# A planned order in which GpSimd waits for VectorE at their shared SBUF port

## The chip, the cores and the metric

The kernel runs on one core of a Trainium2 chip. The metric is device time of one execution in microseconds (us), the median of several runs; lower is better. The engines are called TensorE (PE, its weight loads PEld), VectorE (DVE), ScalarE (ACT), GpSimd (POOL) and SyncE (SP), as in the profile.

## The reference, cut to what matters

Linear attention with a decaying state (batch 4, 8 heads, 768 steps, head size 48), then a Fourier mix of its output and a two-layer network with weights 384 x 1536 and 1536 x 384:

```python
for t in range(S):
    cur = einsum('bhd,bhe->bhde', u * k[t], v[t])
    y[t] = einsum('bhd,bhde->bhe', r[t], state + cur)
    state = w[t] * state + einsum('bhd,bhe->bhde', k[t], v[t])
...
u = x + real(fft(fft(x, axis=1), axis=2))     # x: y with the heads side by side
un = (u - mean(u)) / sqrt(var(u) + 1e-06)
out = u + relu(un @ w_ch1) @ w_ch2
```

## The kernel before

**The work.** Each of the 4 batches is cut into 6 chunks of 128 steps. A chunk of attention loads `in_w`, `in_k`, `in_r` and `in_v`, takes the logarithm of w (`lb`, ScalarE), sums it up with TensorE, takes exponentials (`e`), scales r and k with them (`rkh`), transposes these (`rkt`), multiplies them into a masked matrix (`ah`), and adds the state's part; `rk` = r\*k\*u, its row sums `dc` and `vtd` = v\*`dc` carry the current step; `x` is the sum (L1060). `vb` is v in bf16 (L969). Then a batch is folded (`sd`, `xf`), mixed by TensorE (`hcs`, `hcr`, `uf`), normalised (`bst`, `agg`, `un`), and passed through the network in two halves: W1 gives `ht` (L1188, evicted by L1193 or L1195), W2 gives `osb` (L1206, L1210), which is stored. The first three pairs of chunks of batch 0 use `attention2`, the other chunks `attention`. The attention of one batch runs beside the network of the one before it.

**The order.** Every operation is made once by `g.op(...)` and has a number, in the order of the calls. Many operations can run on two or three engines (`alts`). `ORDER` gives each engine the list of numbers that it executes, in that order; an operation that is in GpSimd's list runs on GpSimd. Five operations of the list that are spoken of below: 555 is `vb` of chunk 3 of batch 1 (L969), 536 and 537 are two `sd` of batch 1, 538 is an `xf` that reads both, 780 and 781 are `rk` of chunk 5 of batch 1; 252 and 253 are the two requests for W1 and W2.

**The planner.** `schedule` walks the five lists with fixed durations (`alts`), and gives each operation a planned start and end, and each TensorE tile its PSUM bank. It never makes the order. Operations with `o.port` (all on GpSimd but DMA requests, and those of VectorE that are marked `port=("dve",)`: tensor-tensor operations, casts and the like from SBUF to SBUF) are taken as users of one shared port: in the plan, none starts before the last one of the other engine has ended. `emit` then writes the instructions: an instruction waits on semaphores for the operations in its `deps`, which are true data dependences and reuse of buffers and banks. The port has no part in `deps`, so nothing in the program holds two users of the port apart.

Most SBUF tensor-tensor operations come out of the helper `tt` and have its line, L527; `ts` is L531 and L532, `act` L541, `evict` L550 (ScalarE) and L551 (VectorE).

Of the kernel before, what the change touches and what calls it, by code (L numbers as in the profile page):

```python
# [58 lines left out]
    "act": (  # L59
# [12 lines left out]
    "dve": (  # L72
# [15 lines left out]
    "pool": (  # L88
# [11 lines left out]
}  # L100


class _Tile:


    __slots__ = ("bank", "ops", "pool", "n_done", "end")

# [24 lines left out]
class _Prog:  # L132
# [53 lines left out]
    def schedule(self, order):  # L186
# [3 lines left out]
        port = {"dve": 0, "pool": 0}  # L190
# [206 lines left out]
def bass_rwkv6_finch__then__fnet_fourier_mix_kernel(  # L397
# [25 lines left out]
    op = g.op  # L423
# [859 lines left out]
```

How the kernel before makes its waits and increments, by code:

```python
        def run(name, eng):  # L343
            for o in self.order[name]:
                for c, v, d in sorted(o.waits, key=lambda x: x[2].end):
                    eng.wait_ge(sems[c], d.val)
                ins = o.fn(eng)
                if o.sem is not None:
                    ins.then_inc(sems[o.sem], 16)
                elif o.inc:
                    ins.then_inc(sems[name], 1)
            if name == "dve":
                for s in dcount:
                    if s.startswith("out"):
                        eng.wait_ge(sems[s], dcount[s])
                eng.nop()
```

## Time and profile before

| | |
|---|---|
| Median of 3 runs | 191.5 us (191.08 to 192.89) |
| The profiled execution | 190.91 us, of it 189.1 us span |
| Busy: TensorE, its weight loads | 174.9 us (92%), 126.1 us (67%) |
| Busy: VectorE, ScalarE, GpSimd | 161.1 us (85%), 123.5 us (65%), 112.8 us (60%) |
| Loaded and stored | 23.59 MB read, 4.72 MB written |

A share of busy time is a mean over stages that have different limits. A busy TensorE is not one at its peak, since the ends of pipelined matmuls are modelled.

### The profile page before, as it was taken

What the parts mean: (1) busy time and instruction counts of PE and PEld (TensorE: products, weight loads), DVE (VectorE), ACT (ScalarE), POOL (GpSimd) and SP (SyncE); (2) the same over time, 40 slices, a digit from 0 to 9 for tenths busy, and PEclk for the clock granted to TensorE, in tenths of its full rate; (3) what the DMA queues carried; (4) which work ended last, traced back from release to release, by engine and by line L of the source; (5) the groups of instructions that cost most, each with busy time, mean ns of one, the idle gap of its engine ahead of it and who ended that gap; (6) DMA issues with size and microseconds to landing.
All of it is one profiled execution on the core that took longest, in us unless ns stands there. A gap on an engine that the chain in (4) does not pass through costs nothing.

```text
span 189.1 us, 4725 instructions
## 1 busy us (share of the span) xinstructions
PE 174.9 (92%) x1824; PEld 126.1 (67%) x1824; DVE 161.1 (85%) x373; ACT 123.5 (65%) x288; POOL 112.8 (60%) x130
## 2 busy tenths in 40 slices
PE   5899989789995799999999998999999999999993
PEld 2265767456894676766887766765888666787761
DVE  8999999999999989999989978998897585457132
ACT  5889989869997571998799687756464331414200
POOL 2179798987699634989998489985591500000000
PEclk9999999999999999999999999999999999999999
DMA  5999989999999999399896799389321003701214
GB/s 162 325 305 246 196 172 181 182 199 191 189 182 204 200 187 197 79 239 205 191 239 140 150 158 217 61 94 230 62 78 43 3 0 62 224 5 45 83 44 164
DMA packets 102599, 29.00 MB, mean 153 GB/s; under 512 B 98865, under 2 KB 102066, under 8 KB 102450
## 3 DMA queue, kind: packets, MB, share of 16 engines
q1 hardware_dynamic: 102034, 26.36, 64.6%
q0 software_dynamic: 544, 2.36, 6.7%
q8 instruction: 14, 0.23, 0.5%
q14 instruction: 7, 0.06, 0.1%
HBM read 23.59 MB, written 4.72 MB: 150 GB/s over the span
## 4 chain that ended last, share of the span: by engine, by line
PE 50%; DVE 31%; POOL 9%; issue 3%; ACT 3%; DMA 2%; DVEq 0%; POOLq 0%; ACTq 0%
PE bank L1206 18%; PE bank L1188 17%; POOL rk L527 5%; DVE ah L1009 4%; PE bank L1141 3%; DMA rkt<-rkh 2%; PE bank L1118 2%; DVE ah L857 2%; DVE vb L969 2%; POOL rkh L527 2%; DVE rkh L527 2%; DVE rkh L972 2%; DVE x L1060 2%; DVE uf L1143 2%; DVE bst L1147 1%
## 5 line engine op out<-in xcount | busy, mean ns | idle before, releaser
L1188 PE MATMUL bank<-unt,w 128*128 128x384 bf16 x288 | 54.4, 328 | 0.7 <-DVE rkh L972 0.7
L1206 PE MATMUL bank<-w,ht 128*128 128x384 bf16 (+2 forms) x300 | 52.9, 319 | 0.0
L1195 ACT ACTIVATE ht<-bank 128x384 bf16<-128x384 f32 x71 | 32.6, 497 | 21.6 <-PE bank L1188 21.3
L1188 PEld LDWEIGHTS bank<-unt,w 128*128 128x128 bf16 x288 | 38.8, 144 | 7.1 <-DVE rkh L972 1.1
L1206 PEld LDWEIGHTS bank<-w,ht 128*128 128x128 bf16 x300 | 27.8, 98 | 15.2
L527 POOL TENSOR_TENSOR rk<-rk,ub 128x384 f32<-128x384 f32 x22 | 22.7, 1037 | 7.5 <-ACT ub L550 7.0
L1210 DVE SCALAR_TENSOR_TENSOR osb<-bank,rstd,uf 128x384 f32<-128x384 f32 (+2 forms) x25 | 14.5, 594 | 12.7 <-PE bank L1206 11.7
L1009 DVE TENSOR_TENSOR ah<-bank,msk 128x512 bf16<-128x512 f32 x36 | 23.3, 676 | 0.7 <-PE bank L1004 0.4
L527 POOL TENSOR_TENSOR vtd<-in_v,dc 128x384 f32<-128x384 f32 (+1 forms) x24 | 20.2, 846 | 5.0 <-DVE dc L961 3.4
L527 POOL TENSOR_TENSOR rkh<-in_k,e 128x384 bf16<-128x384 f32 x18 | 18.2, 1012 | 4.3 <-ACT e L784 2.0
L527 POOL TENSOR_TENSOR rk<-in_r,in_k 128x384 f32<-128x384 f32 x19 | 20.0, 1059 | 0.9 <-DMA in_k<-in_k_dram 0.9
L541 ACT ACTIVATE un<-uf,agg 128x384 bf16<-128x384 f32 x22 | 13.2, 615 | 10.9 <-DVE agg L1149 10.8
L1193 DVE TENSOR_SCALAR ht<-bank 128x384 bf16<-128x384 f32 x25 | 12.7, 549 | 5.3 <-PE bank L1188 5.2
L550 ACT ACTIVATE rkt<-bank 128x512 bf16<-128x512 bf16 x25 | 15.9, 642 | 1.6 <-PE bank L994 0.9
L527 POOL TENSOR_TENSOR sd<-x 128x385 f32<-128x385 f32 x11 | 11.1, 1008 | 7.8 <-DVE x L1060 5.6
L527 POOL TENSOR_TENSOR xf<-sd 128x384 bf16<-128x384 f32 (+1 forms) x11 | 11.5, 1053 | 4.9 <-DVE sd L527 4.9
L1143 DVE TENSOR_TENSOR uf<-bank,x 128x384 f32<-128x384 f32 x24 | 12.7, 548 | 1.3 <-PE bank L1141 1.1
L1147 DVE BATCH_NORM_STATS2 bst<-uf 128x6 f32<-128x384 f32 x24 | 12.9, 549 | 0.1
L541 ACT ACTIVATE lb<-in_w 128x384 bf16<-128x384 f32 (+1 forms) x21 | 12.0, 572 | 0.9 <-PE bank L947 0.5
L940 ACT ACTIVATE bank<-bank 128x384 f32<-128x384 f32 x18 | 8.5, 485 | 6.1 <-PE bank L934 5.9
L972 DVE TENSOR_TENSOR rkh<-bank,in_r 128x384 bf16<-128x384 f32 x18 | 9.9, 548 | 1.3 <-DMA in_r<-in_r_dram 1.2
L541 ACT ACTIVATE vb<-in_v 128x384 bf16<-128x384 f32 x21 | 10.9, 527 | 0.0
(161 smaller groups left out, 359.1 us busy)
## 6 DMA issues: line engine op xcount, KB each, us to landing
out_dram<-osb SPq DMA_DIRECT2D x23, 192.0 KB, 2.0
in_v<-in_v_dram SPq DMA_DIRECT2D x18, 192.0 KB, 3.9
in_w<-in_w_dram SPq DMA_DIRECT2D x18, 192.0 KB, 4.4
in_r<-in_r_dram SPq DMA_DIRECT2D x18, 192.0 KB, 4.1
in_k<-in_k_dram SPq DMA_DIRECT2D x18, 192.0 KB, 4.1
w<-in_moe_w_ch_dram POOLq DMA_DIRECT2D x2, 1152.0 KB, 9.9
in_r<-in_r_dram SPq DMA_DIRECT2D x3, 384.0 KB, 4.8
in_k<-in_k_dram SPq DMA_DIRECT2D x3, 384.0 KB, 4.8
```

What stands on the lines that cost most here:

```text
L527: return lambda e: e.tensor_tensor(out=o, in0=a, in1=b, op=f)
L541: return lambda e: e.activation(o, a, f, **kw)
L550: {"act": lambda e: e.activation(o(), i(), ACTF.Copy), "dve": lambda e: e.tensor_copy(out=o(), in_=i())}, **kw)
L972: op("dve", v_1(DM), lambda e: e.tensor_tensor(out=rh[:, :, 0:D], in0=ps(tce)[:, 0:DM].rearrange("t (h d) -> t h d", d=D), in1=rt[:, :, :] ...
L1009: masked[n] = op("dve", v_1(512), lambda e, x=x: e.tensor_tensor(out=ah[:, x:H:2, :], in0=ps(ta[x])[:, :].rearrange("p (h t) -> p h t", t= ...
L1143: op("dve", v_1(DM), lambda e, kb=kb, t=t: e.tensor_tensor(out=uf[:, kb, :], in0=ps(t)[:, 0:DM], in1=xb[:, kb, 0:DM], op=ALU.add), r=[t, ( ...
L1147: op("dve", v_1(DM), lambda e, kb=kb, bs=bs: e.bn_stats(bs[:, :], uf[:, kb, :]), r=[("UF", i, kb)], w=[("BST", n % 4)])
L1188: ins = e.matmul(ps(t)[:, 0:384], W1[:, m, j:HID:NJ], unt[:, :, m, :], start=(m == 0), stop=(m == NM - 1))
L1193: {"dve": lambda e, j=j, t=t, ht=ht: e.tensor_scalar(out=ht[:, j, :], in0=ps(t)[:, 0:384], scalar1=-1.0, scalar2=0.0, op0=ALU.mult, op1=AL ...
L1195: "act": lambda e, j=j, t=t, ht=ht: e.activation(ht[:, j, :], ps(t)[:, 0:384], ACTF.Relu, scale=-1.0)},
L1206: ins = e.matmul(ps(t)[:, 0:hi - lo], ht[:, j, 128 * x:128 * x + 128], W2[:, j, lo:hi], start=(j == 0), stop=(j == NJ - 1))
L1210: op("dve", v_1(hi - lo) + 64, lambda e, kb=kb, t=t, o=o, lo=lo, hi=hi: e.scalar_tensor_tensor(out=o[:, lo:hi], in0=ps(t)[:, 0:hi - lo], s ...
```

## The change

In the planner, each GpSimd operation that uses the port gets the last VectorE user of the port that was planned ahead of it (`ahead`) as a dependence, so `emit` writes a semaphore wait for it, unless another wait implies it. In the plan such a GpSimd operation starts no earlier than that operation's end plus GpSimd's latency. The two weight requests become users of the port. VectorE's operations get no new dependence.

The five lists are new: 99 of the 1457 operations run on another engine than before (22 from GpSimd to VectorE, 16 from VectorE to GpSimd, 31 from VectorE to ScalarE, 26 from ScalarE to VectorE, 3 from ScalarE to GpSimd, 1 from GpSimd to ScalarE), and the places within the lists differ. VectorE has 374 operations instead of 373, GpSimd 122 instead of 126, ScalarE 291 instead of 288. By the marks in the code 74 VectorE operations use the port, 66 before. The lists around operation 555, and the code:

```diff
     "dve": (
...
-        "321 339 535 330 532 561 556 593 506 585 555 588 553 398 592 786 564 563 566 595 596 785 404 568 789 570 "
...
+        "477 583 330 532 556 588 535 506 557 584 536 555 537 585 592 553 64 564 563 596 595 568 566 402 786 570 379 "
...
     "pool": (
...
-        "244 250 252 66 196 459 460 261 494 488 489 433 523 517 462 518 491 583 584 557 589 520 253 551 536 552 537 "
-        "780 538 781 554 539 586 569 571 599 601 572 809 838 783 839 867 868 810 873 933 907 870 812 934 841 939 "
...
+        "252 244 249 431 488 494 261 269 283 433 523 517 459 518 460 253 589 489 65 462 520 551 491 552 538 586 554 "
+        "539 569 572 601 602 780 781 809 810 844 873 783 838 812 867 901 907 839 902 868 841 933 870 939 934 1120 "
...
@@ -188,6 +188,7 @@
         at = {e: 0 for e in self.ENGS}
         engt = {e: 0 for e in self.ENGS}
         port = {"dve": 0, "pool": 0}
+        ahead = None
         bank = [None] * 8
...
@@ -220,7 +221,7 @@
                 late = 1
                 if o.port:
 
-                    p = port["pool" if e == "dve" else "dve"]
+                    p = port["pool"] if e == "dve" else ahead.end + self.LAT[e] if ahead else 0
                     late = int(e == "dve" or p <= s)
                     s = max(s, p)
...
@@ -240,6 +241,10 @@
             engt[e] = s + dur
             if o.port:
                 port[e] = s + o.dur
+                if e == "pool" and ahead:
+                    o.deps.add(ahead)
+            if o.port and e == "dve":
+                ahead = o
...
-            asked[n] = op("pool", d, lambda e, T=T, x=x: e.dma_start(T[:, :, :], x), w=[n], sem=n, xfer=f)
+            asked[n] = op("pool", d, lambda e, T=T, x=x: e.dma_start(T[:, :, :], x), w=[n], sem=n, xfer=f, port=("pool",))
```

## Rows read from the trace of the kernel before

**Rows 1.** Busy time of each engine in three stretches: us, count in brackets, clock, DMA share:

```profile
20.00:76.00 56.00, 49.49 (x696) 36.75 (x692) 55.02 (x107) 43.91 (x106) 43.45 (x50) 1.00 0.98 191
76.00:140.00 64.00, 62.90 (x659) 46.96 (x660) 60.06 (x131) 48.99 (x118) 53.18 (x57) 1.00 0.79 155
140.00:189.00 49.00, 46.01 (x317) 33.41 (x314) 26.93 (x58) 14.10 (x36) 4.73 (x5) 1.00 0.22 69
```

**Rows 2.** The chain that ended last: start us, us, what:

```profile
58.03 3.87 DVE vb L969
...
176.88 8.49 PE bank L1206 x64
```

**Rows 3.** Timeline of VectorE: start us, us, line, operation, shapes, count:

```profile
20.17 1.02 DVE L527 TENSOR_TENSOR rkh<-in_k,e 128x384 bf16<-128x384 f32 x1
...
21.92 1.29 DVE L527 TENSOR_TENSOR rk<-in_r,in_k 128x384 f32<-128x384 f32 x1
...
33.19 0.82 DVE L527 TENSOR_TENSOR xf<-x 128x191 bf16<-128x191 f32 x1
...
34.53 1.36 DVE L527 TENSOR_TENSOR rkh<-in_k,e 128x384 bf16<-128x384 f32 x1
35.80 2.23 DVE L527 TENSOR_TENSOR xf<-x 128x192 bf16<-128x192 f32 x2
...
57.95 3.95 DVE L969 CAST vb<-in_v 128x384 bf16<-128x384 f32 x1
...
71.58 1.39 DVE L527 TENSOR_TENSOR rkh<-in_k,e 128x384 bf16<-128x384 f32 x1
```

**Rows 4.** VectorE rows of two lines: ns min/median/max, first and last start us:

```profile
L527 DVE TENSOR_TENSOR xf<-x x4: 395/984/1158, 30.5 to 36.9; 128x192 bf16<-128x192 f32 x2, 128x191 bf16<-128x191 f32 x2
...
L969 DVE CAST vb<-in_v x3: 345/350/3954, 57.9 to 133.2; 128x384 bf16<-128x384 f32 x3
```

**Rows 5.** Timeline of GpSimd from 57.8 to 64 us:

```profile
57.81 1.00 POOL L527 TENSOR_TENSOR sd<-x 128x385 f32<-128x385 f32 x1
...
60.70 0.98 POOL L527 TENSOR_TENSOR rk<-rk,ub 128x384 f32<-128x384 f32 x1
62.91 0.83 POOL L527 TENSOR_TENSOR vtd<-in_v,dc 128x384 f32<-128x384 f32 x1 [1.23 <-DVE dc L961]
```

**Rows 6.** Waits of TensorE: us in total, times, longest us:

```profile
PE bank L988 <- DVE rkh L972: 3.2, 1, 3.2
...
PE bank L1030 <- DVE rkh L527: 0.9, 1, 0.9
```

**Rows 7.** Groups of VectorE by line and form: count, busy us, mean ns:

```profile
L1193 DVE TENSOR_SCALAR ht<-bank 128x384 bf16<-128x384 f32 x25 | 12.7, 549 | 5.3 <-PE bank L1188 5.2
...
L551 DVE COPY rkt<-bank 128x512 bf16<-128x512 bf16 x11 | 4.6, 414 | 0.5 <-PE bank L994 0.4
...
L551 DVE COPY unt<-bank 128x384 bf16<-128x384 bf16 x6 | 2.1, 349 | 0.0
```

**Rows 8.** Timeline of VectorE and GpSimd around 70 us; in brackets idle time and releaser:

```profile
69.71 0.56 DVE L527 TENSOR_TENSOR sd<-x 128x385 f32<-128x385 f32 x1 [0.78 <-POOL sd L527]
70.18 0.55 DVE L527 TENSOR_TENSOR rkh<-in_k,e 128x384 bf16<-128x384 f32 x1
...
70.35 1.25 POOL L527 TENSOR_TENSOR xf<-sd 128x384 bf16<-128x384 f32 x1 [0.68 <-DVE sd L527]
```

**Rows 9.** Waits of all engines and of the SyncE queue: total, times, longest:

```profile
DVE rkh L972 <- DMA in_r<-in_r_dram: 1.2, 1, 1.2
...
SPq L346 <- DVE rkh L972: 7.6, 3, 5.7
```

**Rows 10.** The weight tiles: ns min/median/max of a request, first and last; landing:

```profile
L1206 PE MATMUL bank<-w,ht x300: 219/326/337, 68.8 to 185.7; 128*128 128x384 bf16 x138, 128*128 128x256 bf16 x6, 128*128 128x128 bf16 x6
...
L745 POOL DMA_DIRECT2D w<-in_moe_w_ch_dram x2: 607/793/979, 33.7 to 54.3; - x2
...
DMA to landing us min/median/max: 9.1/9.9/10.8
```

114 rows, old and new, of the table ORDER are left out of this document.

## The prediction

> **What bounds the kernel now.** I read the busy times by stage first. From 20 to 76 us VectorE works 55.0 of 56 us and the DMA engines 0.98 of the time; from 76 to 140 us TensorE works 62.9 of 64 us with VectorE close behind (60.1); after that TensorE alone is full [rows 1]. The chain of waits agrees: up to about 75 us it runs mostly over VectorE, later over TensorE, and it ends in W2's matmuls [rows 2]. TensorE's order is fixed, and the network's matmuls that fill the end can't start before the attention that VectorE feeds. So time that VectorE saves before 76 us moves the end; time saved by GpSimd alone moves nothing. The granted clock is 1.00 in all stages, so TensorE runs at its 2.4 GHz level throughout, and no term of the sum is about the clock.
>
> Second, VectorE's timeline. Single instructions of one form take very different times: the cast `vb` 3.95 us at 57.95 us [rows 3] against 0.35 for its fellows [rows 4]. The reader is to lay GpSimd's timeline beside it: GpSimd runs from 57.81 to 61.68 us without a pause, four operations (`sd`, `rk`, `xf`, `rk`, of which rows 5 have the first and the last), and the cast ends when they do. The next operation of GpSimd had to wait for VectorE [rows 5]. TensorE stood still for 3.2 us in the meantime [rows 6]. A cast that was to be short lost its turn at the port to a queue of GpSimd operations that were in no hurry.
>
> **What the added wait removes.** Stalls of that kind on VectorE between 20 and 76 us, from the timeline [rows 3], each less its undisturbed length (0.55 for a 384-column tensor-tensor operation [rows 8], 0.40 for an `xf` of 192 and 0.35 for the cast [rows 4]): `rkh` 1.02 - 0.55 = 0.47; `rk` 1.29 - 0.55 = 0.74; `xf` 0.82 - 0.40 = 0.42; `rkh` 1.36 - 0.55 = 0.81; two `xf` 2.23 - 0.72 (two of 0.40 that overlap by 0.08) = 1.51; the cast 3.95 - 0.35 = 3.60; `rkh` 1.39 - 0.55 = 0.84. Together 8.4 us. With the wait, a GpSimd operation that the plan puts behind such a VectorE operation can't run before it. For the cast (operation 555) the new lists alone would do: 536 and 537 stand around it on VectorE itself, 538 needs 537, and 780 and 781 come ten places later in GpSimd's list. I take the 8.4 us as removed. What is late next is GpSimd (below) and TensorE: its waits for two of these rows, 3.2 us and 0.9 us [rows 6], are 4.1 us, a second and lower measure of the same gain, since it counts only where TensorE had run dry.
>
> **What the new order adds to VectorE.** Its first 185 places (up to about 76 us) take in from GpSimd 12 tensor-tensor operations of 384 columns, 2 of half size and 2 small fills, and from ScalarE 3 copies of 512 columns, 1 of 384 and 3 `ht`; they give to GpSimd 4 of 384 columns, 3 of half size and 3 fills, and to ScalarE 5 copies of 512 columns, 3 of 384, 1 `hcs`, 2 `ht` and the cast 784. One costs its length less about 0.08 of overlap (0.47 from start to start where the length is 0.56 [rows 8]). In: 12 x 0.47 + 2 x 0.32 + 0.1 + 3 x 0.33 + 0.27 + 3 x 0.47 [rows 4, 7, 8] = 9.1 us. Out: 4 x 0.47 + 3 x 0.32 + 0.2 + 5 x 0.33 + 3 x 0.27 + 0.5 + 2 x 0.47 + 0.27 = 7.2 us. The net 1.9 us lies on VectorE, so on the path. Left: 8.4 - 1.9 = 6.5 us. GpSimd and ScalarE have room for their side (43.5 and 43.9 of 56 us busy [rows 1]).
>
> **What the waits cost.** A GpSimd operation that waits holds all of GpSimd's queue behind it: `vtd`, which VectorE adds to `x`; `rkh`, which TensorE transposes; `rk`, which VectorE sums. After the set-up the new list has VectorE's port users in thirteen groups that GpSimd has work behind, six of them before 76 us, the longest with six and with five operations in a row. No row of before shows such a wait. Its lower end is a true dependence between the two: `sd` ends on VectorE at 70.27 us and GpSimd's `xf` starts at 70.35 [rows 8], 0.08 us a group, 0.5 us for six. Its upper end is that each group makes a product late by a whole GpSimd operation, 1.0 us [rows 5], on the path: 6 us. It could also gain beyond the 8.4 us, since GpSimd is itself delayed at the port now (the `xf` at 70.35 takes 1.25 against 1.0 [rows 5, 8]), but GpSimd is not the bound and I count nothing. I take 2.3 us, two groups that pass on their delay: the two long ones hold GpSimd for over 2 us (5 x 0.47), the others for 0.5 to 1.9, which GpSimd's 12.5 us of idle time [rows 1] can hide. If that cover is gone, the upper end holds.
>
> The Trainium skill (SBUF — State Buffer, "SBUF: two separate sides") says that the shared port pair is an exclusive lock, held for the full instruction, and the loser fully blocks. The trace agrees for the tensor-tensor operations (at most 0.84 us lost, less than one GpSimd operation), not for the cast, which lost 3.60 us to four.
>
> **Weight requests.** They take 0.61 and 0.98 us on GpSimd as before. Each can now wait up to one group of VectorE's operations, and W2's stands about two GpSimd operations earlier in its list. W2 was asked for at 54.3 us and needed 9.1 to 10.8 us; its first matmul is at 68.8 [rows 10]. That is at least 3.7 us of cover, and I cost it at nothing; without the cover, TensorE stands for the whole delay. The reordered loads on SP's queue I cost at nothing too: VectorE's longest wait for a load is 1.2 us, once, while the queue itself waits 7.6 us for VectorE to free buffers [rows 9].
>
> **The sum.** 8.4 - 1.9 - 2.3 = 4.2 us. The profiled execution took 190.91 us (189.1 of span, 1.8 around it), 0.6 below the median of the runs shown. The execution becomes 186.7 us, the median 191.5 - 4.2 = **187.3 us**. With the bounds of the wait's cost it is 185.5 (0.5 instead of 2.3) to 191.0 (6).
>
> **The rivals.**
> 1. All of the stalls go and the waits are free, and the exchanged work finds gaps: 191.5 - 8.4 = 183.1 to 185.5, say 184.8. For it: GpSimd gets 4 operations fewer. Against: nothing is free in a stage that is 98% busy. Chance 0.12.
> 2. The loads become the bound. The DMA engines are busy 0.98 of the 56 us [rows 1], so a stage with the same transfers can shrink by 1.1 us: 190.4. Against: much of what moves before 76 us is loaded ahead and waits for buffers [rows 9]. Chance 0.12.
> 3. The change doesn't do what it says: the wait orders GpSimd behind planned operations only. Where GpSimd runs late, its operations that the plan has ahead still meet VectorE at the port. Then the cast's stall goes by the new lists, and half of the other 4.8 us stays: 187.3 + 2.4 = 189.7. Against: GpSimd idles 12.5 us before 76 us [rows 1], so it is seldom late. Chance 0.07.
> 4. One GpSimd operation is the most that a VectorE operation can lose at the port, and what the cast lost beyond 1.0 us, 2.6 us, has another cause that stays: 187.3 + 2.6 = 189.9. Against: the cast ended just when GpSimd's queue did [rows 3, 5]. Chance 0.04. [...]
> 5. Slower: lock-step. VectorE's list is fixed too, so when GpSimd has waited for a group, its next `vtd` or `rkh` is late, VectorE stands in front of it, and the next group comes later still. The price is 1.0 us a group over all thirteen, as TensorE has only 1.1 us of idle time left from 76 to 140 us [rows 1]; against the 6.5 us it decides from the seventh group on. With ten: 191.5 - 6.5 + 10 = 195.0. Against: GpSimd idles 12.5 us from 20 to 76 us and 10.8 us from 76 to 140 us [rows 1]. Chance 0.13.
>
> **How the numbers follow.** The forecast has 0.52. A difference of 1% (1.9 us) is about what a measurement of this kernel can tell from none. Faster than 189.6: the forecast's 0.52 less 0.04 at its slow end, the first rival's 0.12, and some of the third, 0.04: 0.64. Slower than 193.4: the fifth and a little more, 0.14. The rest, 0.22, lies within 1%. The range is 184.3 to 193.0: it takes in the forecast's 185.5 to 191.0, the second to fourth rivals, most of the first and the mild end of the fifth.
>
> **What the profile after would show.** The cast at about 0.35 us, and no VectorE instruction of L527 over 1.0 us before 75 us; TensorE's 3.2 us wait gone; GpSimd idle with VectorE's L527 or L969 as releaser, which is rare now; VectorE's busy time lower by some 6 us in spite of one more instruction. Wrong: VectorE waiting for GpSimd's `vtd`, `rkh` or `rk` for more than 4 us in all, or for loads; W2's first matmul waiting for its transfer; stalls at the port that stay although the wait is there.

## The result, and the profile after

Median 186.21 us (184.5 to 187.82), beside 191.78 us for the kernel before on the same chip: a ratio of 0.9675, 95% interval 0.9586 to 0.9763. That is 5.6 us less between the medians and 6.2 by the ratio, where 4.2 were forecast. The profiled execution took 186.0 us, 184.2 of it span. Comparisons leave out an execution that is over 1.5% above the fastest of its kernel; of the changed kernel that hits 2 of all 11 (187.82 and 189.13 us).

A correction to the section on the kernel before: counted from 0, operation 555 is `vb` of chunk 4 of batch 1, and 780 and 781 are `rk` of chunk 0 of batch 2. Their lines and times stand. From L527 on, lines after are 5 higher (L527 is L532, L969 is L974, L988 is L993, L745 is L750).

Busy time by engine of the whole span, from the page after; VectorE had 161.1 us before:

```profile
PE 175.2 (95%) x1824; PEld 125.8 (68%) x1824; DVE 155.6 (84%) x374; ACT 123.4 (67%) x291; POOL 105.0 (57%) x126
```

The stages after, in the columns of [rows 1]:

```profile
20.00:76.00 56.00, 55.25 (x764) 41.42 (x762) 54.40 (x120) 49.71 (x119) 45.33 (x54) 1.00 0.98 188
76.00:140.00 64.00, 62.35 (x643) 46.20 (x642) 59.47 (x128) 46.35 (x116) 47.65 (x52) 1.00 0.74 160
```

Read the first figure behind the comma, TensorE. In the same 56 us it works 55.25 us where it worked 49.49 [rows 1]: 5.8 us more. That covers the gain (the two spans differ by 4.9 us), and all of it lies before 76 us: from 76 to 140 us TensorE works 62.35 us where it worked 62.90. VectorE is as full as before, but gets 120 instructions done instead of 107. The DMA engines stay at 0.98.

TensorE's waits after, longest first (total, times, longest):

```profile
PE bank L1232 <- POOL osb L602: 2.1, 1, 2.1
PE bank L1169 <- ACT un L546: 1.2, 2, 1.0
```

The first is in the set-up, which the kernel before has too. The 3.2 us and the 0.9 us of [rows 6] are gone. What was the stalled cast of [rows 3], from VectorE's timeline after:

```profile
56.12 0.81 DVE L532 TENSOR_TENSOR rkh<-in_k,e 128x384 bf16<-128x384 f32 x1
...
57.78 0.35 DVE L974 CAST vb<-in_v 128x384 bf16<-128x384 f32 x1
```

and GpSimd beside it:

```profile
55.49 1.02 POOL L532 TENSOR_TENSOR rk<-rk,ub 128x384 f32<-128x384 f32 x1
58.68 1.00 POOL L532 TENSOR_TENSOR xf<-sd 128x384 bf16<-128x384 f32 x1 [2.18 <-DVE sd L532]
```

GpSimd is idle from 56.5 to 58.7 us, and the cast runs in that gap in 0.35 us. The `rkh` of 0.81 us is the longest stall left in this stage, 0.26 us over its 0.55 of [rows 8]; with three of 0.10 to 0.15 us some 0.7 us remain. So 7.7 of the 8.4 us of [rows 3] are gone from this stage. GpSimd stands idle for VectorE (its waits after, excerpt):

```profile
POOL sd L532 <- DVE sd L532: 8.8, 4, 3.8
...
POOL rk L532 <- DVE rk L532: 2.6, 2, 2.0
...
POOL w L750 <- DVE xf L532: 2.5, 1, 2.5
```

Not all of this is the price of the added waits. Experiment 1 below has the new lists without them, and there GpSimd waits for VectorE's `sd` no less:

```profile
POOL sd L530 <- DVE sd L530: 9.4, 4, 4.2
```

So the first row comes of the lists, and so does the gap around the cast: in experiment 1 GpSimd is idle for 3.46 us there. The row of `w` is the waits' own. Nobody wants that time back: VectorE's longest waits for GpSimd and for loads are

```profile
DVE xf L532 <- POOL sd L532: 1.1, 1, 1.1
...
DVE rkh L977 <- DMA in_r<-in_r_dram: 1.0, 1, 1.0
...
DVE x L1065 <- POOL vtd L532: 0.6, 1, 0.6
```

### The profile page after: what moved, and what is told of

Read it like the earlier page. It is cut to its first block, busy times and chain, and to the rows that moved or that the text cites. A ratio compares the mean times of both kernels' runs of the same rounds, so it can differ in the third digit from the quotient of the medians.

```text
span 184.2 us, 4725 instructions
## 1 busy us (share of the span) xinstructions
PE 175.2 (95%) x1824; PEld 125.8 (68%) x1824; DVE 155.6 (84%) x374; ACT 123.4 (67%) x291; POOL 105.0 (57%) x126
## 4 chain that ended last, share of the span: by engine, by line
PE 53%; DVE 16%; ACT 11%; POOL 6%; SPq 5%; DMA 4%; issue 3%; POOLq 0%; DVEq 0%
PE bank L1211 20%; PE bank L1193 16%; SPq L592 5%; PE bank L1146 4%; ACT rkt L555 2%; PE bank L1123 2%; DMA in_v<-in_v_dram 2%; PE bank L1232 2%; DMA in_w<-in_w_dram 2%; DVE x L1065 2%; DVE rkh L532 2%; POOL rk L532 2%; ACT lb L546 1%; DVE ah L1014 1%; ACT vb L546 1%
## 5 line engine op out<-in xcount | busy, mean ns | idle before, releaser
L1193 PE MATMUL bank<-unt,w 128*128 128x384 bf16 x288 | 55.6, 328 | 0.1
L1211 PE MATMUL bank<-w,ht 128*128 128x384 bf16 (+2 forms) x300 | 54.8, 320 | 0.0
L532 POOL TENSOR_TENSOR rk<-rk,ub 128x384 f32<-128x384 f32 x21 | 21.0, 1006 | 2.8 <-DVE rk L532 2.0
L532 POOL TENSOR_TENSOR vtd<-in_v,dc 128x384 f32<-128x384 f32 (+1 forms) x23 | 19.1, 834 | 2.2 <-DVE dc L966 1.1
L555 ACT ACTIVATE rkt<-bank 128x512 bf16<-128x512 bf16 x28 | 17.2, 637 | 1.7 <-PE bank L999 0.7
L532 POOL TENSOR_TENSOR rk<-in_r,in_k 128x384 f32<-128x384 f32 x17 | 17.1, 1014 | 1.9 <-DMA in_k<-in_k_dram 0.9
L532 POOL TENSOR_TENSOR rkh<-in_k,e 128x384 bf16<-128x384 f32 x16 | 15.9, 1004 | 2.9 <-ACT e L958 1.7
L532 POOL TENSOR_TENSOR xf<-sd 128x382 bf16<-128x382 f32 (+1 forms) x12 | 12.0, 1003 | 8.1 <-DVE sd L532 3.1
L532 POOL TENSOR_TENSOR sd<-x 128x385 f32<-128x385 f32 x8 | 8.1, 1007 | 10.7 <-DVE sd L532 8.8
L546 ACT ACTIVATE un<-uf,agg 128x384 bf16<-128x384 f32 x18 | 10.8, 620 | 3.9 <-DVE agg L1154 3.9
L546 ACT ACTIVATE lb<-in_w 128x384 bf16<-128x384 f32 (+1 forms) x21 | 11.8, 572 | 1.5 <-DMA in_w<-in_w_dram 1.4
L546 ACT ACTIVATE vb<-in_v 128x384 bf16<-128x384 f32 x23 | 11.8, 520 | 1.2 <-DMA in_v<-in_v_dram 1.2
```

Source lines behind the costliest of these rows:

```text
L532: return lambda e: e.tensor_tensor(out=o, in0=a, in1=b, op=f)
L546: return lambda e: e.activation(o, a, f, **kw)
L555: {"act": lambda e: e.activation(o(), i(), ACTF.Copy), "dve": lambda e: e.tensor_copy(out=o(), in_=i())}, **kw)
L1193: ins = e.matmul(ps(t)[:, 0:384], W1[:, m, j:HID:NJ], unt[:, :, m, :], start=(m == 0), stop=(m == NM - 1))
L1211: ins = e.matmul(ps(t)[:, 0:hi - lo], ht[:, j, 128 * x:128 * x + 128], W2[:, j, lo:hi], start=(j == 0), stop=(j == NJ - 1))
```

## The experiments

Theory: VectorE's stalls at the port, above all the one at 58 us, held TensorE up; the waits and the lists take them away. Rivals: the cast's kind is to blame and not the port; the new lists gain by something else; the weight requests or the loads decide. Ratios are to the kernel before on the same chip, with 95% intervals.

**1. The new lists, plan and banks, without the waits**

```diff
-                if e == "pool" and ahead:
-                    o.deps.add(ahead)
```

> The changed kernel with its new lists, its plan and its banks, but without the added waits of GpSimd. Theory (the wait removes the port stalls, the new lists alone remove only the cast's): the cast is short, TensorE's stop of 3.2 us is gone, but tensor-tensor stalls of 0.4 to 0.85 us each come back on VectorE, some 3 to 5 us in all; about 188.5 us. Rival (the new lists do it all, the waits are idle): no stall over 0.3 us comes back; 186.2 us as the changed kernel. Rival (the waits do it all): the cast or another cast stalls for 3 us again; 190 us or more.

186.18 us, 0.9685 (0.9633 to 0.9738). Stalls come back on VectorE; from its timeline:

```profile
33.12 1.45 DVE L530 TENSOR_TENSOR xf<-x 128x191 bf16<-128x191 f32 x1
...
59.24 0.35 DVE L972 CAST vb<-in_v 128x384 bf16<-128x384 f32 x1
...
97.87 1.27 DVE L535 TENSOR_SCALAR un<-uf,agg 128x384 bf16<-128x384 f32 x1
```

The cast meets nobody here, as the prediction said of the new lists. Others do: added up as in the prediction, each instruction less its undisturbed length, VectorE's stalls over the whole span are some 6 us here, 9 before and 2 to 3 after. The longest wait of TensorE for one of their products is 1.0 us in all (L1118 <- `xf`). So most stalls cost little, and the lists alone bring the gain, or all but some 2 us of it (experiments 10 and 11).

**2. The old lists with the waits.** The five lists of before in the changed kernel; the planner, its waits and the requests as port users stay. The plan also gives 230 of the 329 TensorE tiles another PSUM bank than in the kernel before.

```diff
 ORDER = {
...
-        "477 583 330 532 556 588 535 506 557 584 536 555 537 585 592 553 64 564 563 596 595 568 566 402 786 570 379 "
+        "321 339 535 330 532 561 556 593 506 585 555 588 553 398 592 786 564 563 566 595 596 785 404 568 789 570 "
...
```

> The lists of before with the changed planner, so with the added waits and the weight requests as port users. Theory: the 8.4 us of stalls on VectorE before 76 us go, the waits give some 2 us back; 185.5 to 187 us. Rival (the new lists do it): the waits hold GpSimd's queue in an order that was not made for them, and VectorE and TensorE then wait for its vtd and rkh; 191 us or more.

185.92 us, 0.9672 (0.961 to 0.9735). The row of the casts, to be laid beside that of [rows 4]:

```profile
L974 DVE CAST vb<-in_v x3: 342/350/352, 56.5 to 127.3; 128x384 bf16<-128x384 f32 x3
```

The waits bring the gain without the new lists as well. That the new banks are not the reason for most of it is shown by the next experiment, which keeps the banks of before. The two halves of the change don't add up: each removes the same stop.

**3. The kernel before with one wait: 780 behind the cast**

```diff
+    g.ops[780].deps.add(g.ops[555])
     g.schedule(ORDER)
```

The lists and all PSUM banks stay those of the kernel before.

> The kernel before with one wait more: GpSimd's rk of chunk 5 of batch 1 (operation 780) waits for the cast of chunk 3 (operation 555). Theory: the cast can be blocked by one GpSimd operation alone, some 0.9 us, TensorE's stop of 3.2 us shrinks below 0.6 us, and the end moves by it: 191.8 - 2.7 = 189.1 us. Rival (the stop is given back to the loads or to GpSimd's late rk and xf): 191 us or more.

187.62 us, 0.9758 (0.9694 to 0.9822): 2.4 of the 3.3%. VectorE, then GpSimd:

```profile
57.64 1.07 DVE L969 CAST vb<-in_v 128x384 bf16<-128x384 f32 x1
```

```profile
57.47 1.02 POOL L527 TENSOR_TENSOR sd<-x 128x385 f32<-128x385 f32 x1
58.88 1.02 POOL L527 TENSOR_TENSOR rk<-in_r,in_k 128x384 f32<-128x384 f32 x1 [0.39 <-DVE vb L969]
```

The cast waits for the `sd` that had started before it and then gets the port, since `rk` stands back. TensorE's wait at L988 falls from 3.2 [rows 6] to 0.3 us. One wait out of all of them does most of the work, with nothing else changed.

**4. The three casts as a two-operand operation**

```diff
-"dve": lambda e: e.tensor_copy(out=vb[:, :, :], in_=vt[:, :, :])}
+"dve": tt(vb[:, :, :], vt[:, :, :], vt[:, :, :], ALU.max)}
```

> The kernel before with the three VectorE casts of v made as a tensor-tensor operation, max(v, v), with the same value and 0.55 us instead of 0.35. Theory (a cast of one SBUF source does not get the port between two GpSimd operations that follow each other at once, a tensor-tensor operation does): the operation at about 58 us takes 1.5 us at most instead of 3.95, TensorE's stop falls below 1 us, about 189.3 us. Rival (whatever comes to the port then must wait for the whole queue): 3.5 us or more again and 191.8 us.

192.14 us, 0.9991 (0.9951 to 1.0032). Nothing changed but the name in the row:

```profile
58.13 4.13 DVE L527 TENSOR_TENSOR vb<-in_v 128x384 bf16<-128x384 f32 x1
```

The stall is as long without a cast, and TensorE waits 3.3 us for `rkh` at L988. So the cast's kind is not to blame.

**5. As 2, but no wait for the cast**

```diff
-            if o.port and e == "dve":
+            if o.port and e == "dve" and o.idx != 555:
                 ahead = o
```

> The lists of before with the added waits, except that no GpSimd operation waits for the cast of chunk 3 of batch 1 (operation 555). Theory (one stall, the cast's, is most of the gain; the stalls of tensor-tensor operations are worth about 1.5 us): the cast takes 3.5 us or more again, TensorE stops for 3 us, and the time is 190 to 190.5 us. Rival (each stall counts at its length, 4.8 us without the cast's): 187.5 us.

190.11 us, 0.9865 (0.977 to 0.996).

```profile
57.21 3.00 DVE L974 CAST vb<-in_v 128x384 bf16<-128x384 f32 x1
```

The stall is back, at three GpSimd operations instead of four (the fourth, `rk` at 62.54 us, waits 2.55 us for a `rkh` of VectorE), and so is a wait of TensorE of 2.2 us (L993 <- `rkh`). Beside experiment 2 the wait for the cast is worth some 4 of its 6 us, all the others together some 2; this is between two chips, and the interval here is wide.

**6. The kernel before, the cast moved to ScalarE** (555 out of VectorE's list and behind 560 in ScalarE's)

```diff
-... 593 506 585 555 588 553 398 ...
+... 593 506 585 588 553 398 ...
-... 832 400 560 347 779 ...
+... 832 400 560 555 347 779 ...
```

> The kernel before with that one cast (operation 555) on ScalarE, in its list behind the copy of rkt of the same chunk; no wait is added. Theory (whatever takes this cast out of the port's way gives the gain): 187.6 us, as with the one wait. Rival (the gain of the one wait came from holding GpSimd back): 190 us or more.

192.63 us, 1.0112 (0.9957 to 1.0267): no gain. My expectation that any way to take the cast off the port would do fell. VectorE, and GpSimd beside it:

```profile
61.17 4.45 DVE L527 TENSOR_TENSOR rkh<-in_k,e 128x384 bf16<-128x384 f32 x1
```

```profile
60.73 0.99 POOL L527 TENSOR_TENSOR xf<-sd 128x384 bf16<-128x384 f32 x1
61.69 0.99 POOL L527 TENSOR_TENSOR rk<-rk,ub 128x384 f32<-128x384 f32 x1
...
64.38 0.82 POOL L527 TENSOR_TENSOR vtd<-in_v,dc 128x384 f32<-128x384 f32 x1
```

VectorE's next port user in line ran into the same unbroken row of GpSimd operations and lost to five of them (the two left out are `vtd` and `xf`); the row ended there, and so did the stall. TensorE again stood 3.2 us, now for `ah`, which VectorE has behind that `rkh`. The cause is the row of GpSimd operations, not the operation that meets it.

**7. The changed kernel, requests no longer port users**

```diff
-..., w=[n], sem=n, xfer=f, port=("pool",))
+..., w=[n], sem=n, xfer=f)
```

> The changed kernel, but the two weight requests are no users of the port: in the plan nothing waits for them, and they wait for nothing. Theory (they have cover): 186.2 us as the changed kernel, within 1 us. Rival (a request that takes the port holds up VectorE's xf beside it, 0.6 us and more, on the path): 187.5 us.

189.62 us, 0.9922 (0.9877 to 0.9967). Stalls at the port stay away (1 to 2 us over the span), yet most of the gain is lost. First what TensorE waited for, then GpSimd's and SyncE's timelines:

```profile
PE bank L999 <- POOL rkh L532: 5.0, 1, 5.0
```

```profile
31.11 0.98 POOL L750 DMA_DIRECT2D w<-in_moe_w_ch_dram  x1
...
42.23 0.99 POOL L532 TENSOR_TENSOR rk<-in_r,in_k 128x384 f32<-128x384 f32 x1 [6.71 <-DMA in_k<-in_k_dram]
```

```profile
31.11 0.76 SPq L592 DMA_DIRECT2D in_k<-in_k_dram  x1
31.91 0.65 SPq L592 DMA_DIRECT2D in_w<-in_w_dram  x1
32.61 6.06 SPq L592 DMA_DIRECT2D in_k<-in_k_dram  x1
```

The first request goes out at 31.11 instead of 33.86 us, since its wait of 2.5 us for VectorE is gone. SyncE asks for the `in_k` that this `rk` reads at 31.11 us too, and it lands only with the weights' 1152 KB. Its size and time to landing here, and then in the changed kernel, where it is asked for at 31.16 us, 2.7 us ahead of the request:

```profile
in_k<-in_k_dram SPq DMA_DIRECT2D x1, 192.0 KB, 11.0
```

```profile
in_k<-in_k_dram SPq DMA_DIRECT2D x1, 192.0 KB, 4.1
```

GpSimd stands 6.7 us in front of its `rk`, and TensorE 5.0 us behind that. The load that takes 6.06 us to be issued is a later `in_k`; it lands at 43.6 us, after this `rk` has started, so the expectation of experiment 9 names the wrong load. In experiment 1 the same wait is missing, but there the request left at 32.17 us, the `in_k` in question had been asked for at 29.99 us and landed after 4.0 us.

**8. The cast with two input tensors: a miss.** The edit hit a `vb` that runs on ScalarE, so the program was in effect the kernel before.

> The kernel before with that one cast made as max(v, k) of two different tensors; this leaves out the true value of v for the state of one chunk. Theory A (an operation that reads two different tensors gets the port at the first end of a GpSimd operation, as rkh and rk did; one that reads a single tensor doesn't): the operation takes 1.5 us at most. Theory B (it depends on what stands ahead of it on VectorE or on GpSimd): about 4.1 us again.

192.8 us in a single run, cast 3.94 us, TensorE's wait 3.1 us: a repeat of [rows 4, 6], and no word on the question.

**9. As 7, the first request two places later, still without a wait** (the banks as in 7)

```diff
     g.schedule(ORDER)
+    q = g.order["pool"]
+    i = q.index(g.ops[252])
+    q.insert(i + 2, q.pop(i))
```

> The changed kernel with the weight requests taken out of the planner's port, as in the run with free requests (its only missing wait that matters is that of the first weight request, line 750, for VectorE's xf: there the request went out at 31.11 us instead of 33.86), but with that request put two places later in GpSimd's queue, behind the two xf operations that follow it. It still waits for nothing itself; the xf operations in front of it start at 33.41 us there, so it goes out near 34.5 us. Theory A (the 5.0 us stop of TensorE with free requests was a transfer that took the DMA engines ahead of the in_k load which SyncE issued at 32.61 us and which then took 6.06 us to issue; only the request's time matters): in_k issued in under 2 us, GpSimd's 6.7 us wait for it and TensorE's 5.0 us stop gone, 186.0 us, 185 to 187.5. Theory B (the wait itself matters, since it keeps GpSimd's port user apart from VectorE's): the stop stays without the wait, 189.5 us.

184.5 us, 0.9598 (0.9554 to 0.9643). GpSimd's timeline:

```profile
34.49 0.98 POOL L750 DMA_DIRECT2D w<-in_moe_w_ch_dram  x1
35.49 1.02 POOL L532 TENSOR_TENSOR rk<-rk,ub 128x384 f32<-128x384 f32 x1
36.46 1.01 POOL L532 TENSOR_TENSOR rk<-in_r,in_k 128x384 f32<-128x384 f32 x1
```

`rk` follows without a pause: the stop is gone, without any wait of the request. Its time was what mattered, not its holding off from the port. (The profiled execution took 189.08 us; it has the loss shown next.)

**10 and 11. The changed kernel, and experiment 1, again on one chip**

> The changed kernel itself, beside the next run on one chip, for the worth of its waits where its own lists stand. The prediction priced them at 2.3 us lost (bounds 0.5 to 6): by that term this run is slower than the next by some 2 us. By the theory that formed after the single runs (GpSimd waits in time that nobody wants of it), both are within 0.5 us of each other, near 186 us.

> The changed kernel's lists, plan and banks without the waits, on the same chip as the run before it. By the prediction's price of the waits 184 us, some 2 us under the run before; by the theory that the stalls of some 6 us that come back on VectorE here, and the waits that GpSimd is spared, both fall into slack: 186 us, within 0.5 us of the run before. If the stalls cost what they take, 190 us or more.

The changed kernel: 184.49 us, 0.9581 (0.9532 to 0.963). The lists without the waits: 186.35 us, 0.9716 (0.9674 to 0.9758). So here the waits gain about 2 us; in the first pair (186.21 and 186.18 us, different chips) nothing. In neither do they cost any, and that they gain was in neither expectation.

The profiled execution of 10 is the one of 189.13 us. What VectorE and then TensorE waited for in it, and SyncE's timeline:

```profile
DVE rk L532 <- DMA in_r<-in_r_dram: 3.3, 1, 3.3
```

```profile
PE bank L1193 <- DVE unt L556: 3.0, 1, 3.0
```

```profile
46.30 1.84 SPq L592 DMA_DIRECT2D in_r<-in_r_dram  x1
```

`in_r` is asked for at 46.30 us, the second request follows at about 47.3, and the slowest `in_r` of the stretch lands after 10.5 us. In the profile of 186.0 us the same load is asked for at 45.06 us and VectorE doesn't wait for it. So 1.2 us decide whether it gets through ahead of the transfer.

**12. The changed kernel, the second request one place later** (as in 9, with 253 and `i + 1`)

> The changed kernel with the second weight request (line 750, at 47.34 us in its profile) one place later in GpSimd's queue, behind the rkh operation after it (49.22 us, 0.99 us long): it goes out near 50.2 us. Theory L (some executions of the changed kernel lose 3 us because the in_r load that SyncE issues at 46 us is caught by this transfer: in the second run's profile it landed after 10.5 us, VectorE waited 3.3 us for it and TensorE 3.0 us): the load gets through before the transfer, no execution stays 3 us over the others, the median is 184 to 185 us, and the weights, landing at 59.5 instead of 57 us, cost the matmuls of line 1211 (first at 58.5 us) at most 1.3 us. Theory M (those executions have another cause, or the later transfer only catches the next load): some execution is again near 189 us, or the median is over 186.

184.66 us, 0.9652 (0.9608 to 0.9695); six executions from 184.41 to 185.19, where the changed kernel's eleven went from 182.96 to 189.13. The request leaves at 49.62 us, `in_r` is asked for at 45.12 us and lands after 4.0 us, VectorE's wait for it is gone, and the price is

```profile
PE bank L1211 <- DMA w<-in_moe_w_ch_dram: 0.3, 1, 0.3
```

The late executions fit the load that the transfer catches. This is not shown to be cured: six executions are too few, and in the profiled one the load was asked for as early as in the changed kernel's profile of 186.0 us. The median is no better than the changed kernel's, so no version here beats it.

## Why the prediction was right, and where its steps were off

**The mechanism** was right: a port user of VectorE that loses to GpSimd operations in no hurry, TensorE standing behind it. The stall went, the wait of TensorE went, the stage before 76 us gave the gain, and VectorE's busy time fell by 5.5 us (161.1 to 155.6) where some 6 were expected. Experiment 6 sharpens it: the cast was only the one that was met. The number is partly luck: the sum took some 4 us too much for the stalls and some 4 us of costs that did not come (both below).

**Stalls, 8.4 us.** As a count it held (7.7 gone). As a price it was too high: experiment 1 keeps some 6 us of them and is as fast as, or 2 us slower than, the changed kernel. The prediction's second and lower measure, the 4.1 us that TensorE waited for two of these rows [rows 6], was the better price: one wait alone (experiment 3) brought 2.4%, 4.6 us, of which the spans of the two profiles, both at full clock, show 3.9 (189.1 to 185.2).

**Exchanged work, +1.9 us.** Not to be seen in the time. The old lists with the waits (0.9672) are not faster than the new ones with them (0.9675, 0.9581).

**Cost of the waits, 2.3 us with bounds of 0.5 to 6.** This is the term that was mis-sized, and that makes the sum too small. Measured on one chip the waits gain some 2 us, on another pair nothing; both lie under the lower bound. I took two of six groups to pass their delay on. GpSimd does stand for long, in good part by the lists alone, but VectorE waits for GpSimd's products only 1.7 us in all, and TensorE hardly. And below nothing I had excluded a gain, since GpSimd isn't the bound; yet the same wait spares VectorE some 4 us of the stalls that experiment 1 has. That this is where the 2 us come from is argued, not shown.

**Requests at nothing.** In the sum that came out right, but the cover I named was not the reason. Without the waits on the requests the kernel is 3.4 us slower (experiment 7 against the changed kernel, 189.62 and 186.21, on two chips), because the first request's wait lets a load go ahead. W2's cover of 3.7 us had shrunk too: its request left at 47.34 us, 7 us earlier than before, but its first matmul came at 58.5 instead of 68.8 us [rows 10]; with the longest transfer of the two, 10.0 us, that leaves 1.2 us.

**Clock at nothing.** The prediction read 1.00 in the one profile. Of the kernel before the run lists have 55 executions with their mean clock. Four are at 1.00 and took 190.3 to 190.8 us (a fifth, of 972.74 us, is left out); 28 are at 0.99, with a median of 191.8; 16 are at 0.98, with one of 193.1. Ten of the changed kernel's eleven have 0.997 or more. So the terms were read from one of the few executions at full clock, and some 1 us of the 5.6 goes with the clock. That is an estimate from these lists; no experiment changed the clock alone.

**The rivals.** The first (stalls go, waits free: 184.8 us) has the waits right; it and the forecast have the same mechanism, and the two medians of the changed kernel, 186.21 and 184.49 us, don't decide between 187.3 and 184.8. The second, loads as the bound, doesn't hold for the median, but decides single executions of the changed kernel (experiment 10). The third: it needs 2.4 us of stalls before 76 us, and some 0.7 stayed. The fifth, lock-step, is excluded by the same chip's pair. The fourth, that one GpSimd operation is the most that can be lost, falls: the long stalls (instructions of 3.95, 4.13, 3.00 and 4.45 us) lost 3.60, 3.58, 2.65 and 3.90 us to three to five, and when the queue behind was made to stand back, the loss was the rest of one operation (0.72 us) and TensorE's wait went with it (experiment 3). The Trainium skill (SBUF — State Buffer, "SBUF: two separate sides") has the loser blocked for the holder's whole instruction; experiment 3 agrees, and the long stalls show that the blocking need not end with that instruction.

**Open:** at which boundary between two GpSimd operations VectorE gets the port. The four long stalls (the kernel before, experiments 4, 5 and 6) end only when GpSimd's row ends. Others end at the first boundary while GpSimd goes on, such as this `rkh` of experiment 3; GpSimd's `rk` begins beside it and then takes 1.33 instead of 1.0 us:

```profile
60.35 0.93 DVE L527 TENSOR_TENSOR rkh<-in_k,e 128x384 bf16<-128x384 f32 x1
```

```profile
59.85 1.01 POOL L527 TENSOR_TENSOR xf<-sd 128x384 bf16<-128x384 f32 x1
60.81 1.33 POOL L527 TENSOR_TENSOR rk<-rk,ub 128x384 f32<-128x384 f32 x1
```

It is the same operation (the `rkh` after that cast) that lost 3.90 us in experiment 6. So it is neither the cast nor the number of inputs; nothing here tells what else decides. That the two engines meet at the port is not shown by a run either: the runs show that a row of GpSimd operations holds a VectorE operation up, and that a wait which opens the row ends it.

## What to carry to other kernels

Price a stall on a full engine by what the last engine in line waits for it, not by its length: here some 4 of 8 us counted, and one added dependence gave most of the gain. Before moving the victim elsewhere, look at who follows it: the next user of the port takes its place, so it is the other side's unbroken row that has to be opened. And where a wait also shifts a large transfer, check which small load is asked for just before and just after it; here a request 2.7 us earlier cost some 3 us, over half of the gain. And read the clock in the list of all executions, not in one profile.

## What the runs showed of the hardware that I had not expected

A VectorE operation of 0.35 to 0.55 us can lose the port to five GpSimd operations in succession and then takes 4.45 us, though none of these begins more than 0.05 us off the end of the one before.

While a weight transfer of 1152 KB asked for by GpSimd is under way, one load of 192 KB (once two) takes SyncE 4.3 to 7.6 us to issue where most take 0.6 to 1.5, and the loads caught by it land after 8.7 to 11.8 us instead of 4 to 5 (the kernel before, the changed kernel, experiments 1, 7, 9, 10, 11 and 12, both transfers of each).

After TensorE's stop of 5.0 us in experiment 7 the granted clock fell, from its 2.4 GHz level to a mean between its two levels; the stage before and the stage after the stop began:

```profile
36.00:42.00 6.00, 3.22 (x33) 2.07 (x31) 4.74 (x10) 2.78 (x7) 0.00 (x0) 1.00 1.08 209
42.00:48.00 6.00, 3.77 (x33) 2.66 (x34) 1.26 (x5) 3.21 (x7) 5.77 (x7) 0.72 0.93 183
```

The clock is the third figure from the end, 1.00 and then 0.72. The changed kernel, without such a stop, has 1.00 in both stages shown above. A stop of some 3 us does not always do it: the kernel before has 1.00 throughout in its profile with a stop of 3.2 us, while experiment 4, whose stop of 3.3 us ended at about 62.7 us, has a mean of 0.51 from 62 to 68 us, close to the 1.2 GHz level:

```profile
62.00:68.00 6.00, 5.13 (x35) 3.11 (x36) 4.55 (x10) 1.83 (x5) 2.89 (x3) 0.51 1.06 212
```
